# The fused attention and expert kernel: keys' blocks moved ahead of the key products, the gate's weight work gathered into four later steps, and two of three weight roundings given to GpSimd

## What is computed

```python
k_n = k / (np.linalg.norm(k, axis=-1, keepdims=True) + 1e-06)
for t in range(S):
    y[:, :, t] = np.einsum('bhd,bhde->bhe', q[:, :, t], state)
    v_old = np.einsum('bhde,bhd->bhe', state, kt)
    state = state + bt[..., None] * np.einsum('bhd,bhe->bhde', kt, vt - v_old)
```

## Time and profile before

| | us |
|---|---|
| median of 3 runs | 1170.54 (1169.98 to 1171.93) |
| the profiled execution | 1170.35 |
| its span in the profile | 1168.6 |
| preparation | 0 to 77 |
| recurrence | 77 to 278 |
| second and third layer | 278 to 1168.6 |

### The profile page before, as it was taken

One profiled execution on the slowest core, in us unless ns is written; L12 is line 12 of the kernel. 1 busy time (PEld: TensorE's weight loads), 2 busy tenths in 40 slices (PEclk: granted clock), 3 DMA queues, 4 the chain that ended last, 5 costly groups with the idle time before them and its releaser, 6 DMA issues.

```text
span 1168.6 us, 29044 instructions
## 1 busy us (share of the span) xinstructions
PE 1116.6 (96%) x11562; PEld 1069.0 (91%) x11562; DVE 647.9 (55%) x1552; ACT 462.5 (40%) x1048; POOL 355.3 (30%) x378
## 2 busy tenths in 40 slices
PE   4898999899999999999999999999999999999996
PEld 3886787778999999999999999999999999999995
DVE  4989788663455646465565647533534343434342
ACT  1236665784333333433333345423333333333331
POOL 4289995542002021020202012322222232322223
PEclk9999999999999999999999999999999999999998
DMA  7553556855997011110101011472424242424221
GB/s 158 127 126 93 132 120 155 220 159 199 370 358 241 21 48 41 35 41 20 41 20 41 15 50 65 172 231 76 165 74 173 76 168 84 157 97 145 62 70 53
DMA packets 82603, 137.30 MB, mean 117 GB/s; under 512 B 11050, under 2 KB 70034, under 8 KB 81466
## 3 DMA queue, kind: packets, MB, share of 16 engines
q1 hardware_dynamic: 68490, 87.97, 25.9%
q0 software_dynamic: 12992, 28.75, 7.6%
q10 hardware_dynamic: 1008, 18.97, 4.3%
HBM read 81.96 MB, written 53.77 MB: 116 GB/s over the span
## 4 chain that ended last, share of the span: by engine, by line
PE 74%; DVE 1%; issue 0%; ACT 0%; POOL 0%; ACTq 0%; POOLq 0%
PE ps_x L1409 18%; PE ps_x L1499 18%; PE ps_h L1398 17%; PE ps_h L1477 17%; PE ps_r L1457 2%; PE ps_r L1448 2%; DVE hg L1817 0%; ACT hg L1607 0%; POOL out_dram L1364 0%; DVE w_parts L1780 0%; PE ps_r L1516 0%; DVE x_raw L1810 0%; PE ps_r L1426 0%; ACT yT_d L1625 0%; PE ps_r L1424 0%
## 5 line engine op out<-in xcount | busy, mean ns | idle before, releaser
L1499 PE MATMUL ps_x<-hg,w_parts 128*128 128x400 f32 x1152 | 230.2, 346 | 0.0
L1409 PE MATMUL ps_x<-w_parts,hg 128*128 128x400 f32 x1152 | 229.7, 346 | 0.0
L1398 PE MATMUL ps_h<-xg,w_parts 128*128 128x384 f32 x1152 | 222.3, 338 | 0.0
L1477 PE MATMUL ps_h<-xg,w_parts 128*128 128x400 f32 x1116 | 220.6, 345 | 1.1 <-DVE w_parts L1780 1.1
L1409 PEld LDWEIGHTS ps_x<-w_parts,hg 128*128 128x128 f32 x1152 | 209.6, 188 | 0.0
L1817 DVE SCALAR_TENSOR_TENSOR hg<-ps_h,hg 128x400 fp32r<-128x400 f32 x128 | 73.6, 575 | 243.1 <-ACT hg L1607 242.6
L1398 PEld LDWEIGHTS ps_h<-xg,w_parts 128*128 128x128 f32 x1152 | 204.0, 188 | 2.5 <-DVE elu_parts L1674 2.5
L1477 PEld LDWEIGHTS ps_h<-xg,w_parts 128*128 128x128 f32 x1116 | 202.7, 188 | 4.0 <-issue 3.1
L1499 PEld LDWEIGHTS ps_x<-hg,w_parts 128*128 128x128 f32 x1152 | 206.0, 188 | 0.0
L1344 POOL DMA_INDIRECT xs_scratch<-x,rows_now x48 | 49.2, 1025 | 393.5 <-DVE rows_now L1754 293.9
L1607 ACT ACTIVATE hg<-ps_h 128x400 fp32r<-128x400 f32 x128 | 64.6, 505 | 256.4 <-PE ps_h L1477 256.4
(11 more groups left out here) (175 smaller groups left out, 1312.4 us busy)
## 6 DMA issues: line engine op xcount, KB each, us to landing
xs_scratch<-pads SPq DMA_DIRECT2D x2, 5502.0 KB, 42.4
x_rows<-xs_scratch SPq DMA_DIRECT2D x17, 614.1 KB
kqT<-in_kqT_dram SPq DMA_DIRECT2D x48, 192.0 KB, 4.0
carried<-in_w_dram ACTq DMA_DIRECT2D x3, 3072.0 KB, 10.9
w_raw<-in_w_dram ACTq DMA_DIRECT2D x3, 3072.0 KB, 11.3
xs_scratch<-pads SPq DMA_DIRECT2D x6, 1375.5 KB, 17.0
out_dram<-pads SPq DMA_DIRECT2D x1, 4800.0 KB, 30.3
xs_scratch<-pads SPq DMA_DIRECT2D x6, 786.0 KB, 8.9
```

The lines of the kernel that those rows point to most:

```text
L1398: mm = nc.tensor.matmul(ps_h[f % 2][:, 0:TB], wi[:, a, k, f * P:(f + 1) * P], xr[:, b, k, :], start=(i == 0), stop=(i == len(passes) - 1))
L1409: mm = nc.tensor.matmul(ps_x[t][:, 0:DG], act_r[:, f % RING, a, t * P:(t + 1) * P], wo[:, b, f, :], start=(f == 0 and i == 0), stop=(f == ...
L1477: mm = nc.tensor.matmul(ps_h[f % 2][:, 0:TR], w1, xg[:, b, k, :], start=(m == 0), stop=(m == len(passes) - 1))
L1499: mm = nc.tensor.matmul(ps_y[k][:, 0:TR], w2r[i][:, a, s, k * P:(k + 1) * P], hg[:, s % RING, b, :], start=(s == 0 and m == 0), stop=(s == ...
```

## The change

Four things are done.

- `diagonal_blocks(0)` reads its keys from `kT` too. SP loads `kT` for i = 0 and 1 first, then moves beta, then loads i = 2 and 3 and after that `kqT[0]`, beta and `kqT[1]`.
- The four key products of chunks 0 and 1 follow `diagonal_blocks(3)` to `(6)`. They are no longer masked by DVE: ACT copies them out of PSUM (`take_products`, two copies each) and GpSimd multiplies the copies with the masks in place.
- `gate_work` starts at i = 8 with four output chunks at each i up to 11 (`GATE_FROM`, `W_CHUNKS`), in place of two at each i from 5 to 12. DVE turns to the second group's norms after 8 columns in place of 12, and ACT takes the root for them behind its copy of output chunk 1. One `keep_clock(256)` before pair 0 is gone.
- In pairs 8 to 11 ACT rounds the first of the three pieces only; GpSimd rounds the second and third with a copy of its own ahead of each subtraction.

```diff
-PREPARED = 12
+PREPARED = 8
+GATE_FROM = 8
+W_CHUNKS = 4
         def chunks_with(i):
-            at = 2 * (i - KT_BUFS - 1)
-            return (at, at + 1) if at >= 0 else ()
+            at = W_CHUNKS * (i - GATE_FROM)
+            return range(at, min(at + W_CHUNKS, FT1)) if at >= 0 else ()
...
+            load_kT(0)
             load_kT(1)
-            for n in range(2):
-                sp.wait_ge(kqT_cleared, n + 1)
-                load_kqT(n)
...
             load_kT(2)
-            for i in range(3, KT_BUFS + 1):
-                sp.wait_ge(chunk_done, i - 2)
-                load_kT(i)
+            load_kT(3)
+            sp.wait_ge(kqT_cleared, 1)
+            load_kqT(0)
             sp.wait_ge(beta_moved, 48)
             sp.dma_start(beta_sb[:].rearrange("p s i -> p (s i)"), beta_turned).then_inc(beta_loaded, 16)
+            sp.wait_ge(kqT_cleared, 2)
+            load_kqT(1)
...
+            pool.wait_ge(masks_cleared, 1 + 2 * (NR - 1 + 2))
+            for n in range(2):
+                for c in range(2):
+                    for h in range(2):
+                        pool.wait_ge(grams_taken, (2 * n + c) * 2 + h + 1)
+                        nc.gpsimd.tensor_tensor(kept_keys(n, c, h), kept_keys(n, c, h), mask_of_keys(), ALU.mult
+                                                ).then_inc(masked, 1)
...
-                        pool.wait_ge(w_hi, i + 1)
+                        if i % W_EACH == 0:
+                            pool.wait_ge(w_hi, i // W_EACH + 1)
+                        else:
+                            pool.wait_ge(w_loaded[i], 16)
+                            if piece.start >= WI_COLS:
+                                pool.wait_ge(gate_set, 1)
+                            nc.gpsimd.tensor_copy(wio[:, 0, piece], w_raw[:, piece]).then_inc(w_rounded, 1)
+                            pool.wait_ge(w_rounded, i - i // W_EACH)
...
             for i in range(NIT // 2):
-                if i < 4:
-                    products_of_keys(i // 2, i % 2)
                 diagonal_blocks(i)
+                if 0 <= i - 3 < 4:
+                    products_of_keys((i - 3) // 2, (i - 3) % 2)
                 gate_work(i)
-            gate_work(NIT // 2)
...
+            def take_products(n, c):
+                act.wait_ge(grams_done, 2 * n + c + 1)
+                for h in range(2):
+                    nc.scalar.activation(kept_keys(n, c, h), of_keys(h).rearrange("p g a s t -> p g a (s t)"), ACT.Copy
+                                         ).then_inc(grams_taken, 1)
...
-                if i == 4:
+                take_blocks(i)
+                if i == 3:
                     root_of(0)
-                if i == 8:
-                    root_of(1)
-                take_blocks(i)
+                if 0 <= i - 3 < 4:
+                    take_products((i - 3) // 2, (i - 3) % 2)
                 for f in chunks_with(i):
                     take_turned(f)
-            for f in chunks_with(NIT // 2):
-                take_turned(f)
+                    if f == 1:
+                        root_of(1)
...
+                if now and m >= W_PAIR:
+                    round_weights((m - W_PAIR) * W_EACH)
                 if now:
-                    round_next()
                     take_solved(a, 1)
-                    round_next()
                     take_solved(b, 1)
-                    round_next()
                     take_solved(a, 2)
...
-            mask_products(0, 0)
-            mask_products(0, 1)
-            mask_products(1, 0)
-            mask_products(1, 1)
```

More of the change, by code:

```diff
@@ L172, in attention_outputs @@
         grams_done = sem("grams_done_a")
+        grams_taken = sem("grams_taken")
         masked = sem("masked")
@@ L192, in attention_outputs @@
         gate_set = sem("gate_set")
-        w_loaded, w_hi, w_split = sems("w_loaded", len(W_CUTS) - 1), sem("w_hi"), sem("w_split")
+        w_loaded, w_hi = sems("w_loaded", len(W_CUTS) - 1), sem("w_hi")
+        w_rounded, w_split = sem("w_rounded"), sem("w_split")
         products_cleared = sem("products_cleared")
@@ L201, in of_keys, with kept_keys, mask_of_keys @@
             return ps_g[h].rearrange("p (g a s t) -> p g a s t", g=2, a=QP // 2, s=2)
+        def kept_keys(n, c, h):
+            return lq[n % KEPT].rearrange("p (g a h) s t -> p g a h (s t)", g=2, h=2)[:, :, c * QP // 2:(c + 1) * QP // 2, h]
+        def mask_of_keys():
+            return masks[:].rearrange("p g s t -> p g (s t)").unsqueeze(2).to_broadcast([P, 2, QP // 2, 2 * P])
         def heads(h):
@@ L322, in _ @@
             load_kT(2)
-            for i in range(3, KT_BUFS + 1):
-                sp.wait_ge(chunk_done, i - 2)
-                load_kT(i)
+            load_kT(3)
+            sp.wait_ge(kqT_cleared, 1)
+            load_kqT(0)
             sp.wait_ge(beta_moved, 48)
             sp.dma_start(beta_sb[:].rearrange("p s i -> p (s i)"), beta_turned).then_inc(beta_loaded, 16)
-            for i in range(KT_BUFS + 1, NIT // 2):
+            sp.wait_ge(kqT_cleared, 2)
+            load_kqT(1)
+            for i in range(KT_BUFS, NIT // 2):
                 if i == NIT // 3:
@@ L444, in diagonal_blocks @@
             def diagonal_blocks(i):
[L446 to L450, removed]
+                pe.wait_ge(kT_loaded[i % KT_BUFS], i // KT_BUFS * 32 + 32)
+                if i:
                     pe.wait_ge(blocks_taken, i)
@@ L457, in diagonal_blocks @@
                         for h in range(2):
[L458 to L461, removed]
+                            k_u = kT[heads(h), i % KT_BUFS, ca // QP, a, rows_of(r)]
                             mm = nc.tensor.matmul(ps_d[rows_of(to), h, ca * BLK:(ca + 1) * BLK], k_u, k_u,
@@ L490, in gate_work @@
                         pe.wait_ge(wgn_loaded, 16)
-                        pe.wait_ge(masked, 8)
+                        pe.wait_ge(grams_taken, 8)
                     turn_output_weights(f)
@@ L501, in products_of_keys @@
                     pe.wait_ge(products_cleared, 1)
+                elif n < 2:
+                    pe.wait_ge(grams_taken, (2 * n + c) * 2)
                 else:
@@ L607, in _ @@
             pe.wait_ge(from_lanes, 1)
-            keep_clock(256)
             keep_clock(256)
@@ L779, in _ @@
                 now, past, more = m < PAIRS, m > 0, m < PAIRS - 1
-                pieces = [(m - W_PAIR) * W_EACH + i if m >= W_PAIR and now else None for i in range(W_EACH)]
-                def round_next():
-                    i = pieces.pop(0)
-                    if i is not None:
-                        round_weights(i)
                 if past:
@@ L909, in mask_products @@
                 for h in range(2):
-                    to = lq[n % KEPT].rearrange("p (g a h) s t -> p g a h (s t)", g=2, h=2)[:, :, c * QP // 2:(c + 1) * QP // 2, h]
-                    nc.vector.tensor_tensor(to, of_keys(h).rearrange("p g a s t -> p g a (s t)"),
-                                            masks[:].rearrange("p g s t -> p g (s t)").unsqueeze(2).to_broadcast([P, 2, QP // 2, 2 * P]),
+                    nc.vector.tensor_tensor(kept_keys(n, c, h), of_keys(h).rearrange("p g a s t -> p g a (s t)"), mask_of_keys(),
                                             ALU.mult).then_inc(masked, 1)
```

2 lines of the change are left out of this document (removed).

## The result

| | before | after |
|---|---|---|
| time, median | 1170.54 us (1166.29 to 1172.00) | 1181.3 us (1175.75 to 1183.26) |
| ratio | | 1.0092, interval 1.0069 to 1.0115 |
| profiled execution, its span | 1170.35, 1168.6 | 1181.3, 1179.6 |
| ACT places the first inverses | 76.91 | 84.77 |
| the second layer's first piece | 278.67 | 289.49 |

The change makes the kernel 0.9% slower, 10.8 us. The forecast was 3.4 us slower, at most 8.5. The network is as long as before: its first piece now starts at 289.49 (it stood at 278.67 in the earlier trace rows), 10.8 us later. So the loss lies ahead of it: in these two executions 7.9 us ahead of pair 0 and 3 us in the recurrence. The first row is from the chain of work that ended last.

The account below looks back on a forecast made before the run. PE bounds the kernel, and in the preparation its instruction fetches set the pace. Pair 0 starts 3.5 us later and pairs 8 to 11 give 0: 1170.35 plus 3.5 is 1173.9 us, range 1165.5 to 1179.0.

Parts of the forecast that it names:

- packets of 127 matmuls: PE's instructions, fetched by DMA in 16 KB packets of 127 or 128 matmuls; PE stops when they run out.
- the eight crossings: Packet boundaries PE meets from 6.3 us until i = 8 is done, each costing one restart interval; 37.0 us in sum.
- the bare fetches: Instruction fetches before i = 8, no longer covered by output chunks, with only four products of 16 between the blocks.
- E: Time PE is done with i = 8: 44.6 us forecast, bounds 35.6 and 51.6; pair 0 starts 35.8 us later.
- quiet fetches: Rival: key loads don't hold up packets, eight fetches of 3.5 us; 5.5 us gained, 1164.9 us; chance 0.14.
- fetch is free: Rival: instruction fetches cost PE nothing, E near 33.5; 7.6 us gained, 1162.7 us; chance 0.03.
- No change: Rival: eight restart intervals average 4.2 us, pair 0 starts at 77.0; 1170.4 us; chance 0.27.
- every fetch is loaded: Rival: key loads meet all eight fetches, 5.5 us each; 10.5 us lost, 1180.8 us; chance 0.14.
- L: Time from one PE restart to the next: 3.5 us with quiet DMA engines, 5.5 with loaded ones.
- Now which L?: Passage sorting the eight fetches before i = 8: four at 5.5, one at 4.5, three at 3.5; sum 37.0 us.
- DVE's wait for the root: Before the second group's reciprocal, DVE was to idle some 4 us until released by ACT's root.
- The last third: Roundings moved from ACT to GpSimd in pairs 8 to 11: taken as 0; bounds 1.5 us gained, 0.7 lost.

Follow-up runs that it names:

- e12: e5 with SP's waits for the key buffers on ACT's copy of the blocks instead of PE's end; 1176.39 us, ratio to before 1.0040.
- e5: The changed kernel with both `kqT` loads taken out of the first batch, issued after the blocks of steps 1 and 2; 1177.65 us, ratio to before 1.0044.
- e3: The changed kernel with v of steps 2 and 3 loaded before SP's wait for the last turned output chunk; 1178.58 us, ratio to before 1.0070.
- e4: The kernel before with v of steps 2 and 3 loaded before SP's wait for the last turned output chunk; 1168.61 us, ratio 0.9985.
- e1: The kernel before with the change of pairs 8 to 11 alone (GpSimd rounds pieces two and three); 1171.49 us, ratio 1.0012.
- e7: The kernel before with the edits of e4 and e1 together; 1169.15 us, ratio 0.9991.
- e8: The changed kernel with `GATE_FROM` 7 instead of 8 and the edits of e3 and e5; 1175.42 us, ratio to before 1.0031.

## Why the prediction was right or wrong

**Right: what bounds, and the direction.** The network moved as a whole, and the start of pair 0 carried most of it. The packets of 127 matmuls, the eight crossings up to i = 8, the first block near 5.2 us and the bare fetches were as worked out. From E on 36.2 us passed, 35.8 were forecast; groups of four chunks ran at their 1.82 us each. e12 is nearly the forecast's own case: with windows of 37.1 us in sum the inverses are placed at 81.4, for 80.4 forecast. The rivals "quiet fetches" and "fetch is free", the latter by the Trainium skill's page Runtime: NRT & Kernel Launch, section Instruction fetch mechanics, which calls the crossing mostly hidden, fall with the 7.32 us stop. "No change" took 4.2 us for every interval; they measured 5.1 on average. The rival "every fetch is loaded" gave nearly the time measured, 1180.8, but not its mechanism: three of the eight windows were at 3.4 to 4.0 us and one at 9.86, and pair 0 started 7.9 us later, not 10.5, in this execution. That the time agrees is luck.

**Failed step 1: L was capped.** "Now which L?" took 5.5 us for every loaded fetch, by windows of before in which at most a few loads were under way, and counted only how many fetches would be loaded. Yet the same paragraph had worked out 3.3 MB and 17 us of transfers from one batch: a packet that queues behind them waits for the rest of the batch, and that is what happened (17.68). The term was mis-sized: 4 x 5.5 for the first three and the sixth, which measured 4.55, 9.86, 6.30 and 5.27, 26.0 in all; with the other four (15.0 for 15.0) the sum is 41.0 for 37.0. Removing loads from the batch gave 3.0 us of these 4.0 back in the sum of the windows (e5), 3.9 with later waits (e12), and 0.48% of the time (e5). The time fell by more than the placing did (84.77 to 82.59), so the profiled execution of after may well be one with an early placing.

**Failed step 2: a chain not looked at.** The prediction compared PE's and DVE's chains to pair 0 and stopped there. The move of the last output chunk also moves what SP has queued behind its wait for it, k and then v of steps 2 and 3, and those release GpSimd. "What is queued behind the wait" was asked of GpSimd's new wait, not of this old one. It brought DVE's waits of 1.07 and 1.77 us where there had been 0.91 and 0.84. Undoing it took 0.22% off after (e3, intervals overlap) and 0.15% off before (e4), so this chain had bound the recurrence before the change as well, and what the change adds by it is about 1 us. The rest of the 3.0 us between 7.9 and 10.8 stays open; the stretch of low clock at 182.4 us and fetch stops that differ between executions lie in it, and e3, placed 10.1 us later than before, says that the preparation can cost that much as well.

**A size: DVE's wait for the root** was 1.22 us, where some 4 were expected, since DVE came late itself. Its norms of the first group ran beside GpSimd's masks (below). It was off the path.

**The last third** was put at 0, and it gave nothing (e1: 1.4 us lost, 0.2 to 2.6; e7 against e4: 0.7.) The casts took 1.04 us, below the 1.5 assumed.

**The sum in hindsight,** for the two profiled executions: 3.5 as forecast, 4.0 for the loaded fetches, above all the second, 0.4 for E + 36.2, together 7.9; 2.9 in the recurrence, in part by GpSimd's chain; 10.8.

## What to carry to other kernels

Loads issued in one batch ahead of need are not free for the engines whose instructions come over the same DMA engines: where PE runs short instructions, place the packets of instructions among the loads and ask how many bytes stand ahead of each. When a piece of work is moved, go through every queue that waits for its end, SP's above all, to the engine that these loads release. Time taken from an engine that nobody waits for is worth nothing, so look for who waits before moving work.

## What the runs showed of the hardware

**A packet of instructions can wait for the whole backlog of loads.** It stood 6.9 us between a restart (10.82) and its start (17.68), with 3.2 MB issued of which 1.4 MB had not moved at the restart; 1.1 us where no load was under way (43.77 to 44.89).

**Some of DVE's operations took longer beside GpSimd's, others did not.** GpSimd's masks, two at a time:

```profile
31.40 2.49 POOL L430 TENSOR_TENSOR carried<-carried,masks 128x512 f32<-128x512 f32 x2 [16.11 <-ACT carried L746]
34.20 2.50 POOL L430 TENSOR_TENSOR carried<-carried,masks 128x512 f32<-128x512 f32 x2 [0.31 <-ACT carried L746]
```

and DVE beside them, with one of the same lines later, when GpSimd is idle:

```profile
31.46 1.29 DVE L869 TENSOR_TENSOR inversion<-inversion 128x64 f32<-128x64 f32 x1
32.78 1.19 DVE L873 TENSOR_TENSOR inversion<-inversion 128x64 f32<-128x64 f32 x1
...
34.24 0.55 DVE L880 RECIPROCAL inversion<-inversion 128x64 f32<-128x64 f32 x1
...
52.30 0.23 DVE L869 TENSOR_TENSOR inversion<-inversion 128x64 f32<-128x64 f32 x1
```

The operations of 64 columns on two operands took about as long as one mask and ended with it, to 0.1 us; such an operation takes 0.23 us alone. The reciprocal beside a mask took the 0.55 us that it takes at 51.71. DVE's columns, with one operand in PSUM, aren't slowed either: 0.52 us in before (at 37.74), where GpSimd is idle, and the same in e8, first beside a mask (GpSimd 40.20 to 42.70), then beside GpSimd's columns:

```profile
40.85 0.52 DVE L247 TENSOR_TENSOR inversion<-inversion,psum 128x350 f32<-128x350 f32 x1
...
72.01 0.52 DVE L247 TENSOR_TENSOR inversion<-inversion,psum 128x350 f32<-128x350 f32 x1
```

That the number and the place of the operands make the difference is an inference from these rows; no run varied them. The Trainium skill, SBUF — State Buffer, section SBUF: two separate sides, has it as a rule: a VectorE operation with two inputs in SBUF and a GpSimd one that reads SBUF exclude each other for a whole instruction. The rows agree, with 1.19 to 1.29 us in place of 0.23.
